# The last 512 tokens of a chained kernel: kept by token, stored by SyncE in place of GpSimd's indirect stores

## The chip, the cores and the metric

One core of a Trainium2 chip runs the whole kernel. The metric is the device time of one execution in microseconds; the median of three runs counts.

## What is computed

Three stages follow each other, each fed by the one before (B 4, H 8, S 768, D 48; 3072 tokens of 384 features):

```
# 1 linear attention with a decay for each key feature
for t in range(S):
    state = alpha[:, :, t, :, None] * state + einsum('bhd,bhe->bhde', k[:, :, t], v[:, :, t])
    y[:, :, t] = einsum('bhd,bhde->bhe', q[:, :, t], state)
x = y.transpose(0, 2, 1, 3).reshape(B * S, H * D)
# 2 each token goes through the one expert of 8 with the highest probability
logits = normed(x) @ normed(expert_emb).T / tau
expert_idx = argmax(logits, axis=1); gate_w = softmax(logits)[expert_idx]
for e in range(8):
    h = maximum(x[mask] @ w1[e], 0)              # 384 -> 1024
    out[mask] = gate_w[mask, None] * (h @ w2[e]) # 1024 -> 384
# 3 a dense network
h = x @ w_in                                     # 384 -> 2048
y = maximum(0.01 * h, h) @ w_out                 # 2048 -> 384
```

## The kernel before

The program is written by hand for the five engines. Each has its own list of instructions (`@block.sync`, `@block.gpsimd`, `@block.scalar`, `@block.vector`, `@block.tensor`), and semaphores order them. Nothing else sets an order: an engine does its instructions in the order written, and a wait holds back all that stands behind it on that engine.

**Attention** runs over 24 tiles of 128 tokens (6 chunks of each of the 4 batches, the batches in turn). SyncE stores each tile's result in the scratch tensor `x_rows` in memory (line 408).

**Routing.** VectorE works out, for every token, the expert and a place: the tokens are sorted by expert, and each expert's tokens begin a new block of 128 slots. 31 blocks (`WINDOWS`; "window" in the code) are enough for every split. Tables for the slots come out of it: `slot_src` (which token sits in a slot), `slot_gate` (its gate), `slot_dst` (the row of `y_rows` to which the slot's result goes), and `wtab`, a number for each block that tells the expert and when weights are to be split. `slot_dst` is worked out at lines 1093 to 1103, behind the splits of expert 0's weights and ahead of the block loop: it takes the empty slots out, so that `y_rows` holds the 3072 results without gaps, sorted by expert. Empty slots get a number beyond the rows and aren't written.

**The block loop** (`each_window`, 31 steps, two for each turn of a hardware loop, the last three written out). In step w TensorE does the hidden layer of block w+1, transposes the hidden values of block w (`hT`), transposes the gathered rows of block w+2 and contracts block w (line 1372). Every product of two fp32 operands is done as three matmuls on a high and a low part (`PARTS`): ScalarE copies the high part (`gxT`, `hT`, `wts`), VectorE subtracts it to get the low part (lines 1066, 1128, 375). VectorE scales the block's result by the gates into `ys` (line 1148), two buffers. GpSimd gathers block w+3's rows out of `x_rows` (line 578), copies the block's token numbers into column 384 of `ys` (line 598), copies its `slot_dst` (line 573), waits for `ys` and scatters the rows into `y_rows` by an indirect DMA (line 603). SyncE loads the next expert's weights (`load_expert`) each time a half of the buffer `raw` has been split.

**The second network** takes `y_rows` in 6 groups of 512 rows. SyncE loads a group in four DMAs, one for each 32 partitions (`load_y`, line 485), when the blocks that can hold its rows have been scattered; VectorE transposes it (line 1110), and TensorE does for each of 16 slices of 128 hidden features `inner` (line 1399) and `outward` (line 1434). ScalarE copies the four tiles of 128 results of a group to `os` (line 780, `o_copy`). As the rows are sorted by expert, the token number that stands beside each row is needed to store it: SyncE loads these numbers once (`tokens`, line 495), and GpSimd stores each tile by an indirect DMA to `out` (line 614), and waits for all stores at the end (line 618).

Each engine leaves the program through the end of the block; the records of this stand under line 64, where the block's context is opened.

## Time and profile before

| | before |
|---|---|
| median of 3 runs | 858.06 us |
| the runs | 859.18, 858.06, 854.04 us |
| the profiled execution | 856.75 us |
| its span, first to last instruction | 855.0 us |
| mean granted TensorE clock | 0.991 |
| TensorE busy (matmuls) | 833.1 us, 97% of the span |
| VectorE / ScalarE / GpSimd busy | 419.2 / 342.7 / 185.7 us |

The profiled execution is one of its own; 1.75 us of it lie outside the span. Attention takes up to about 122 us of the span, routing up to 144.8, the block loop up to about 443, the second network the rest.

### The profile page before, as it was taken

What the parts mean: (1) busy time and instruction counts of PE and PEld (TensorE: products, weight loads), DVE (VectorE), ACT (ScalarE), POOL (GpSimd) and SP (SyncE); (2) the same over time, 40 slices, a digit from 0 to 9 for tenths busy, and PEclk for the clock granted to TensorE, in tenths of its full rate; (3) what the DMA queues carried; (4) which work ended last, traced back from release to release, by engine and by line L of the source; (5) the groups of instructions that cost most, each with busy time, mean ns of one, the idle gap of its engine ahead of it and who ended that gap; (6) DMA issues with size and microseconds to landing.
All of it is one profiled execution on the core that took longest, in us unless ns stands there. A gap on an engine that the chain in (4) does not pass through costs nothing.

```text
span 855.0 us, 17220 instructions
## 1 busy us (share of the span) xinstructions
PE 833.1 (97%) x5554; PEld 751.6 (88%) x5555; DVE 419.2 (49%) x644; ACT 342.7 (40%) x663; POOL 185.7 (22%) x267
## 2 busy tenths in 40 slices
PE   7999999999999999999999999999999999999994
PEld 7888878999989999999999888898999888899993
DVE  7799969625444435445265433433533533433330
ACT  2455547535534435445254333333333323333231
POOL 6566624132223222232120001001001001001001
PEclk9899999999999999999999999999999999999997
DMA  9999761634335242396002201201201001001001
GB/s 211 230 220 222 185 213 56 223 113 163 140 110 193 76 148 102 115 242 205 24 3 38 38 1 38 37 1 37 37 0 37 0 0 38 1 1 37 1 1 37
DMA packets 46677, 76.38 MB, mean 89 GB/s; under 512 B 19559, under 2 KB 35987, under 8 KB 46640
## 3 DMA queue, kind: packets, MB, share of 16 engines
q1 hardware_dynamic: 40976, 60.30, 26.4%
q0 software_dynamic: 5504, 15.59, 5.2%
q8 instruction: 21, 0.34, 0.2%
q14 instruction: 16, 0.13, 0.0%
q10 hardware_dynamic: 160, 0.01, 0.0%
HBM read 61.68 MB, written 15.60 MB: 90 GB/s over the span
## 4 chain that ended last, share of the span: by engine, by line
PE 92%; DVE 2%; DMA 2%; POOL 1%; issue 1%; ACT 0%; SPq 0%; DVEq 0%; POOLq 0%; ACTq 0%
PE bank L1399 24%; PE bank L1434 23%; PE bank L1372 15%; PE bank L1352 15%; PE bank L1363 3%; PE bank L1236 2%; PE bank L1196 2%; PE bank L1213 2%; DMA qkas<-qka 2%; PE bank L1339 1%; PE bank L1244 1%; PE bank L1202 1%; PE bank L1256 1%; POOL kt L536 0%; PE bank L1187 0%
## 5 line engine op out<-in xcount | busy, mean ns | idle before, releaser
L1399 PE MATMUL bank<-yT,wts 128*128 128x512 f32 x864 | 217.0, 395 | 0.0
L1434 PE MATMUL bank<-wts,gs 128*128 128x384 f32 x1152 | 215.0, 334 | 0.0
L1434 PEld LDWEIGHTS bank<-wts,gs 128*128 128x128 f32 x1152 | 202.3, 188 | 8.9 <-issue 0.3
L1399 PEld LDWEIGHTS bank<-yT,wts 128*128 128x128 f32 x864 | 160.7, 188 | 30.7
L1162 DVE TENSOR_TENSOR g<-bank,small 128x512 f32<-128x512 f32 x96 | 66.4, 691 | 172.5 <-ACT small L789 172.5
L1352 PE MATMUL bank<-wts,gxT 128*128 (+1 forms) x558 | 141.5, 398 | 0.6 <-DVE gxT L1074 0.6
L1372 PE MATMUL bank<-wts,hT 128*128 x744 | 137.2, 339 | 0.0
L789 ACT ACTIVATE small<-bank 128x512 f32<-128x512 f32 x96 | 57.6, 600 | 187.5 <-PE bank L1399 180.0
L1372 PEld LDWEIGHTS bank<-wts,hT 128*128 128x128 f32 x744 | 128.5, 188 | 0.2
L1352 PEld LDWEIGHTS bank<-wts,gxT 128*128 128x128 f32 x558 | 101.9, 188 | 19.8 <-issue 0.8
L614 POOL DMA_INDIRECT out<-os,tokens x24 | 23.4, 973 | 377.0 <-ACT os L780 371.5
L1164 DVE TENSOR_TENSOR gs<-g,gs 128x512 fp32r<-128x512 f32 x96 | 66.6, 693 | 67.1 <-ACT gs L792 67.1
L792 ACT ACTIVATE gs<-g 128x512 fp32r<-128x512 f32 x96 | 60.7, 632 | 72.8 <-DVE g L1162 72.8
L748 ACT ACTIVATE hT<-bank 128x512 fp32r<-128x512 f32 x62 | 33.7, 597 | 123.9 <-PE bank L1363 123.9
L375 DVE TENSOR_TENSOR wts<-raw,wts 128x1024 f32 (+1 forms) x60 | 70.1, 1220 | 19.3 <-ACT wts L369 19.3
L603 POOL DMA_INDIRECT y_rows<-ys,idst x31 | 31.6, 1018 | 189.6 <-DVE ys L1148 189.6
L1128 DVE TENSOR_TENSOR hT<-bank,hT 128x512 fp32r<-128x512 f32 x62 | 39.9, 686 | 50.5 <-ACT hT L748 50.2
L369 ACT ACTIVATE wts<-raw 128x1024 f32 (+1 forms) x60 | 59.2, 1058 | 0.0
L1148 DVE TENSOR_SCALAR ys<-bank,slot_gate 128x384 f32<-128x384 f32 x31 | 19.0, 614 | 43.4 <-PE bank L1372 43.4
L720 ACT ACTIVATE hs<-bank 128x512 f32<-128x512 f32 x62 | 37.1, 599 | 4.9 <-PE bank L1352 4.9
L1066 DVE TENSOR_TENSOR gxT<-bank,gxT 128x384 fp32r<-128x384 f32 x30 | 16.7, 558 | 42.0 <-ACT gxT L716 42.0
L578 POOL DMA_INDIRECT xg<-x_rows,isrc x28 | 29.5, 1055 | 25.0 <-POOL isrc L573 24.1
(174 smaller groups left out, 732.9 us busy)
## 6 DMA issues: line engine op xcount, KB each, us to landing
raw<-w SPq DMA_DIRECT2D x14, 1536.0 KB, 7.0
qkas<-qka SPq DMA_DIRECT2D x40, 289.5 KB, 5.0
vs<-v SPq DMA_DIRECT2D x24, 192.0 KB, 4.9
x_rows<-xs SPq DMA_DIRECT2D x24, 192.0 KB, 4.4
yl<-y_rows SPq DMA_DIRECT2D x24, 192.0 KB
raw<-w_in SPq DMA_DIRECT2D x2, 1536.0 KB, 7.0
raw<-w_out SPq DMA_DIRECT2D x2, 1536.0 KB, 7.2
raw<-w SPq DMA_DIRECT2D x3, 512.0 KB, 4.0
```

The costliest lines, as they stand in the source:

```text
L369: act.activation(set_of(par, 0, cols), raw[:, cols], ACT.Copy).then_inc(w_hi, 1)
L375: dve.tensor_tensor(set_of(par, 1, cols), raw[:, cols], set_of(par, 0, cols).bitcast(F32), ALU.subtract).then_inc(w_lo, 1)
L720: act.activation(hs[:, u, half * HALF:(half + 1) * HALF], hps[u][half][:, :], ACT.Relu).then_inc(relu_done, 1)
L789: act.activation(small[:, f % 2], gps[f % 2][:, :], ACT.Copy, scale=0.01).then_inc(small_done, 1)
L792: act.activation(gs[:, f % 4, 0], g[:, f % 2], ACT.Copy).then_inc(g_hi, 1)
L1128: dve.tensor_tensor(hT[:, 1, h], htps[half][:, :], hT[:, 0, h].bitcast(F32), ALU.subtract).then_inc(ht_lo, 1)
L1162: dve.tensor_tensor(g[:, f % 2], gps[f % 2][:, :], small[:, f % 2], ALU.max).then_inc(g_done, 1)
L1164: dve.tensor_tensor(gs[:, f % 4, 1], g[:, f % 2], gs[:, f % 4, 0].bitcast(F32), ALU.subtract).then_inc(g_lo, 1)
L1352: m = pe.matmul(hps[u][half][:, :], gxT[:, u, x_part, k * P:(k + 1) * P], set_of(par, w_part, slice(n, n + HALF)), start=(k == 0 and (x_pa ...
L1372: m = pe.matmul(yeps, hT[:, h_part, k * P:(k + 1) * P], set_of(par, w_part, slice(n, n + D)), start=(k == 0 and (h_part, w_part) == (0, 0) ...
L1399: m = pe.matmul(gps[f % 2][:, :], wts[:, 0, w_part, n:n + P], yT[:, u, y_part, k], start=(k == 0 and (w_part, y_part) == (0, 0)), stop=(k ...
L1434: m = pe.matmul(ops[tt], gs[:, f % 4, g_part, tt * P:(tt + 1) * P], wts[:, 1, w_part, f * D:(f + 1) * D], start=(f == 0 and (g_part, w_par ...
```

## The change

The tokens of the last chunk of each batch, 4 tiles of 128, are called late (`LATE_TILES`: tiles 5, 11, 17 and 23 of the output). The other 2560 (`EARLY`) are treated as before: their rows lie in `y_rows` without gaps, sorted by expert, and make up groups 0 to 4. The late ones get the row `EARLY` + token, so that the scratch tensor has 5632 rows, of which the upper 3072 hold 512 that are written. Group 5 is loaded from those, tile by tile, so its rows are in the order of the output. SyncE then stores the four results of group 5 with plain DMAs, and waits for all stores in GpSimd's place.

`slot_dst` needs more for it: the count of early tokens of each expert (seven small operations, `kept` to `back_by`, between two splits of expert 0's weights), and for every slot whether it is late (`place_slots`, eleven operations, in VectorE's first block, behind the low part of block 2). VectorE's first two blocks are written out ahead of its loop (`each_window(dve, step, 1)`). GpSimd's wait for `slot_dst` moves into the step, behind the gather. The diff leaves out the new tiles and the new semaphore, the shape of `tokens` (20 columns), a condition in `wait_scattered` that leaves out a wait for nothing in blocks 0 and 1, and the size of the scratch tensor.

```diff
@@ -56,10 +56,15 @@
     YW = y_dram.shape[1]
-    assert YW == D + 4
-    y_blk = y_dram[:, 0:D].rearrange("(g n r) (j d) -> g j r n d", r=SQ, j=QUADS, n=GT // SQ)
-    y_token = y_dram[:, D:YW].rearrange("(t p) d -> p t d", p=P)
+    EARLY, LATE_TILES = N - GT, [b * CH + CH - 1 for b in range(BATCHES)]
+    Y_ROWS = EARLY + N
+    assert YW == D + 4 and y_dram.shape[0] == Y_ROWS and TG == BATCHES
+    y_blk = y_dram[0:EARLY, 0:D].rearrange("(g n r) (j d) -> g j r n d", r=SQ, j=QUADS, n=GT // SQ)
+    y_late = y_dram[EARLY:, 0:D].rearrange("(t n r) (j d) -> t j r n d", r=SQ, j=QUADS, n=P // SQ)
+    y_token = y_dram[0:EARLY, D:YW].rearrange("(t p) d -> p t d", p=P)
+    o_rows = out.rearrange("(t p) d -> t p d", p=P)
@@ -333,9 +341,11 @@
-        def each_window(eng, step):
-            with eng.Fori(0, WINDOWS // 2 - 1) as i:
+        def each_window(eng, step, apart=0):
+            for w in range(2 * apart):
+                step(w, w % 2, True, True)
+            with eng.Fori(apart, WINDOWS // 2 - 1) as i:
                 for u in range(2):
@@ -475,13 +486,18 @@
-                newest = min(t * TG + TG - 1 + E - 1, WINDOWS - 1)
+                newest = min(t * TG + 2 * TG - 1 + E - 1, WINDOWS - 1)
                 for j in range(2):
                     sp.wait_ge(scattered[j], 16 * ((newest + 2 - j) // 2))
                 if t >= 2:
                     sp.wait_ge(yt_turned, (t - 1) * KD)
                 for j in range(QUADS):
+                    if t == GROUPS - 1:
+                        for tt, tile in enumerate(LATE_TILES):
+                            sp.dma_start(yl[j * SQ:(j + 1) * SQ, u, tt * P // SQ:(tt + 1) * P // SQ],
+                                         y_late[tile, j]).then_inc(yl_in[u], 16)
+                        continue
                     sp.dma_start(yl[j * SQ:(j + 1) * SQ, u],
@@ -495,6 +511,12 @@
                 load_y(t, t % 2)
+            for tt, tile in enumerate(LATE_TILES):
+                sp.wait_ge(o_copied, (GROUPS - 1) * TG + tt + 1)
+                sp.dma_start(o_rows[tile], os_[:, 1, tt]).then_inc(late_stored, 16)
+            for u, s in enumerate(stored):
+                sp.wait_ge(s, 16 * TG * (GROUPS // 2 - u))
+            sp.wait_ge(late_stored, 16 * TG)
@@ -586,7 +608,6 @@
             pool.wait_ge(id_space, 1)
-            pool.wait_ge(tables_ready, 3)
@@ -595,6 +616,7 @@
                 wait_scattered(pool, w, u, pool_turns)
+                pool.wait_ge(tables_ready, 3)
                 pool.tensor_copy(ys[:, u, D:D + 1].bitcast(I32), slot_src[:, ds(w, 1)]).then_inc(idx_copied, 1)
@@ -602,20 +624,18 @@
                     out=y_dram, out_offset=bass.IndirectOffsetOnAxis(ap=idst[:, u:u + 1].bitcast(U32), axis=0),
-                    in_=ys[:, u, :], in_offset=None, bounds_check=N - 1, oob_is_err=False).then_inc(scattered[u], 16)
+                    in_=ys[:, u, :], in_offset=None, bounds_check=Y_ROWS - 1, oob_is_err=False).then_inc(scattered[u], 16)
             each_window(pool, step)
             pool.wait_ge(tokens_in, 16)
-            for t in range(GROUPS):
+            for t in range(GROUPS - 1):
                 for tt in range(TG):
                     n = t * TG + tt
                     pool.wait_ge(o_copied, n + 1)
                     pool.indirect_dma_start(
                         out=out, out_offset=bass.IndirectOffsetOnAxis(ap=tokens[:, n, 0:1].bitcast(U32), axis=0),
                         in_=os_[:, t % 2, tt], in_offset=None, bounds_check=N - 1, oob_is_err=False).then_inc(stored[t % 2], 16)
-            for s in stored:
-                pool.wait_ge(s, 16 * TG * (GROUPS // 2))
@@ -1034,8 +1054,6 @@
             tok, clear, empty, far, ghi = (slot_val[:, j, :] for j in range(5))
-            more = exp8[:, 6, 0:E - 1]
-            start("side", dve.tensor_tensor(more, base[:, 1:E], base[:, 0:E - 1], ALU.subtract))
             dve.wait_ge(slots_summed, 1)
@@ -1087,26 +1105,29 @@
             split_lo(dve, 0, 0, range(3, 4))
+            kept, kept_sum, kept_from, back, limit, back_by, limit_by = (exp_early[:, j, :] for j in range(7))
+            start("main", dve.tensor_tensor(kept, incl[:, :, TILES - TG - 1], starts, ALU.subtract))
+            after("main")
+            start("main", dve.tensor_tensor_scan(kept_sum, kept, zeros[:, 0:E], 0.0, ALU.add, ALU.add))
+            start("side", dve.scalar_tensor_tensor(out=limit, in0=cx, scalar=float(P), in1=kept, op0=ALU.mult, op1=ALU.add))
+            after("main")
+            start("main", dve.tensor_tensor(kept_from, kept_sum, kept, ALU.subtract))
+            after("side")
+            start("side", dve.tensor_tensor(limit_by[:, 0:E - 1], limit[:, 1:E], limit[:, 0:E - 1], ALU.subtract))
+            after("main")
+            start("main", dve.scalar_tensor_tensor(out=back, in0=cx, scalar=float(P), in1=kept_from,
+                                                   op0=ALU.mult, op1=ALU.subtract))
+            after("main")
+            start("main", dve.tensor_tensor(back_by[:, 0:E - 1], back[:, 1:E], back[:, 0:E - 1], ALU.subtract))
             gx_rest(1, 1)
             split_lo(dve, 0, 0, range(4, PIECES))
-            start("main", dve.tensor_tensor(wexp[:, :, 0:E - 1], wexp[:, :, 0:E - 1],
-                                            more.unsqueeze(1).to_broadcast([P, W, E - 1]), ALU.mult))
-            after("main")
-            start("main", dve.tensor_reduce(far, wexp[:, :, 0:E - 1], AX.X, ALU.add))
-            after("main")
-            start("main", dve.tensor_tensor(far, slot_row[:, :], far, ALU.subtract))
-            after("main")
-            start("main", dve.tensor_tensor(far, far, empty, ALU.add))
-            after("main")
-            dve.wait_ge(tables_ready, 2)
-            dve.tensor_copy(slot_dst[:, :], far).then_inc(tables_ready, 1)
             dve.wait_ge(gate_ready, 1)
             def y_turn(t, u, k):
                 if k == 0:
-                    dve.wait_ge(yl_in[u], (t - u) * 8 * QUADS + 16 * QUADS)
+                    loads = QUADS * (t // 2 + (TG if t == GROUPS - 1 else 1))
+                    dve.wait_ge(yl_in[u], 16 * loads)
                 dve.transpose(yf[:, (u * KD + k) % 2].rearrange("p (n r) -> p n r", r=SQ),
@@ -1114,6 +1135,39 @@
+            def place_slots():
+                def by_window(ap):
+                    return ap[:, 0:E - 1].unsqueeze(1).to_broadcast([P, W, E - 1])
+                back_w, limit_w, is_late = far, ghi, tok
+                after("main")
+                after("side")
+                start("main", dve.tensor_tensor(by_win[:, :, :], wexp[:, :, 0:E - 1], by_window(back_by), ALU.mult))
+                start("side", dve.tensor_tensor(wexp[:, :, 0:E - 1], wexp[:, :, 0:E - 1], by_window(limit_by), ALU.mult))
+                after("main")
+                start("main", dve.tensor_reduce(back_w, by_win[:, :, :], AX.X, ALU.add))
+                after("side")
+                start("side", dve.tensor_reduce(limit_w, wexp[:, :, 0:E - 1], AX.X, ALU.add))
+                after("main")
+                start("main", dve.tensor_tensor(back_w, slot_row[:, :], back_w, ALU.subtract))
+                after("side")
+                start("side", dve.scalar_tensor_tensor(out=is_late, in0=slot_row[:, :], scalar=limit[:, 0:1], in1=limit_w,
+                                                       op0=ALU.subtract, op1=ALU.is_ge))
+                after("main")
+                start("main", dve.scalar_tensor_tensor(out=clear, in0=clear, scalar=float(EARLY), in1=back_w,
+                                                       op0=ALU.add, op1=ALU.subtract))
+                after("side")
+                start("side", dve.tensor_tensor(back_w, back_w, empty, ALU.add))
+                after("main")
+                start("main", dve.tensor_tensor(clear, clear, is_late, ALU.mult))
+                after("side")
+                after("main")
+                start("main", dve.tensor_tensor(far, far, clear, ALU.add))
+                after("main")
+                dve.wait_ge(tables_ready, 2)
+                dve.tensor_copy(slot_dst[:, :], far).then_inc(tables_ready, 1)
@@ -1129,6 +1183,8 @@
                     gx_rest(w + 2, u)
+                if isinstance(w, int) and w == 0:
+                    place_slots()
                 with dve.If(late > 0):
@@ -1147,7 +1203,7 @@
-            each_window(dve, step)
+            each_window(dve, step, 1)
```

## How the change moves instructions

VectorE ahead of the block loop, before, from the last operation of the table `wtab` on (`exp` is the tile `exp8` with the experts' numbers, `squares` holds the slots' flags by expert, `slot_val` the slots' values):

```order
L1088 CAST wtab<-wflag 1x31
L375 TENSOR_TENSOR wts<-raw,wts 128x1024
L1066 TENSOR_TENSOR gxT<-bank,gxT 128x384
L375 TENSOR_TENSOR wts<-raw,wts 128x1024 x2
L1093 TENSOR_TENSOR squares<-squares,exp 128x31x7
L1096 TENSOR_REDUCE slot_val<-squares 128x31
L1098 TENSOR_TENSOR slot_val<-slot_row,slot_val 128x31
L1100 TENSOR_TENSOR slot_val<-slot_val 128x31
L1103 CAST slot_dst<-slot_val 128x31
L338 UNCONDITIONAL_BRANCH
```

and after:

```order
L1106 CAST wtab<-wflag 1x31
L386 TENSOR_TENSOR wts<-raw,wts 128x1024
L1109 TENSOR_TENSOR exp_early<-incl,exp 128x8
L1111 SCALAR_TENSOR_TENSOR exp_early<-exp_early,zeros 128x8
L1112 SCALAR_TENSOR_TENSOR exp_early<-exp,exp_early 128x8
L1114 TENSOR_TENSOR exp_early<-exp_early 128x8
L1116 TENSOR_TENSOR exp_early<-exp_early 128x7
L1118 SCALAR_TENSOR_TENSOR exp_early<-exp,exp_early 128x8
L1121 TENSOR_TENSOR exp_early<-exp_early 128x7
L1084 TENSOR_TENSOR gxT<-bank,gxT 128x384
L386 TENSOR_TENSOR wts<-raw,wts 128x1024 x2
L356 TENSOR_LOAD wtab
```

The seven operations on `exp_early` now stand ahead of block 1's low part (`gxT`), and the five that gave `slot_dst` are gone from ahead of the loop.

VectorE in block 0, after; before, the first three rows were followed by the branch to the weights' splits:

```order
L1182 TENSOR_TENSOR hT<-bank,hT 128x512 x2
L1084 TENSOR_TENSOR gxT<-bank,gxT 128x384
L1147 TENSOR_TENSOR by_win<-squares,exp_early 128x217
L1148 TENSOR_TENSOR squares<-squares,exp_early 128x31x7
L1150 TENSOR_REDUCE slot_val<-by_win 128x31
L1152 TENSOR_REDUCE slot_val<-squares 128x31
L1154 TENSOR_TENSOR slot_val<-slot_row,slot_val 128x31
L1156 SCALAR_TENSOR_TENSOR slot_val<-slot_row,exp_early,slot_val 128x31
L1159 SCALAR_TENSOR_TENSOR slot_val<-slot_val 128x31
L1162 TENSOR_TENSOR slot_val<-slot_val 128x31
L1164 TENSOR_TENSOR slot_val<-slot_val 128x31
L1167 TENSOR_TENSOR slot_val<-slot_val 128x31
L1170 CAST slot_dst<-slot_val 128x31
```

Eleven operations up to `slot_dst` now stand between block 2's low part and the splits of expert 1's weights.

The end of the list of SyncE before, with the waits:

```order
L485 DMA yl<-y_rows 32x16x96 [waits yt_turned,scattered1,scattered0]
L485 DMA yl<-y_rows 32x16x96 x3
L64 UNCONDITIONAL_BRANCH
```

and after:

```order
L498 DMA yl<-y_rows 32x4x96 [waits yt_turned,scattered1,scattered0]
L498 DMA yl<-y_rows 32x4x96 x15
L516 DMA out<-os 128x384 [waits o_copied] x4
L69 UNCONDITIONAL_BRANCH [waits late_stored,stored1,stored0]
```

and the end of GpSimd's, before and after:

```order
L614 DMA out<-os,tokens 3072x384 [waits o_copied,tokens_in]
L614 DMA out<-os,tokens 3072x384 [waits o_copied] x23
L64 UNCONDITIONAL_BRANCH [waits stored1,stored0]
```

```order
L636 DMA out<-os,tokens 3072x384 [waits o_copied,tokens_in]
L636 DMA out<-os,tokens 3072x384 [waits o_copied] x19
L69 UNCONDITIONAL_BRANCH
```

Four stores and the wait for all stores have gone from GpSimd to SyncE, and the last group's four loads have become sixteen.

## Rows read from the trace of the kernel before

**Rows 1.** The page: busy time, and the chain's shares by engine

```profile
PE 833.1 (97%) x5554; PEld 751.6 (88%) x5555; DVE 419.2 (49%) x644; ACT 342.7 (40%) x663; POOL 185.7 (22%) x267
PE 92%; DVE 2%; DMA 2%; POOL 1%; issue 1%; ACT 0%; SPq 0%; DVEq 0%; POOLq 0%; ACTq 0%
```

**Rows 2.** Chain of waits at the end: start us, us, what

```profile
842.38 0.50 ACT os L780
...
844.88 0.98 POOL out L614
```

**Rows 3.** Records of the program's end: count, duration ns, start us

```profile
L64 SPq DRAIN  x1: 122/122/122, 612.1 to 612.1; - x1
L64 PEldq DRAIN  x1: 3342/3342/3342, 839.0 to 839.0; - x1
...
L64 POOLq DRAIN  x1: 7098/7098/7098, 847.7 to 847.7; - x1
L618 POOLq EVENT_SEMAPHORE  x1: 17/17/17, 847.5 to 847.5; - x1
```

**Rows 4.** GpSimd, order of time: its last store of group 4

```profile
784.79 0.98 POOL L614 DMA_INDIRECT out<-os,tokens  x1 [0.30 <-issue]
```

**Rows 5.** Chain of waits, TensorE in blocks 0 and 1

```profile
147.47 4.16 PE bank L1352 x18
...
154.90 4.19 PE bank L1372 x24
...
164.44 4.19 PE bank L1372 x24
```

**Rows 6.** SyncE's stores of x (line 408): all 24, then the one at 119.6

```profile
DMA to landing us min/median/max: 1.8/4.4/7.6
...
L408 SPq DMA_DIRECT2D x_rows<-xs x1: 344/344/344, 119.6 to 119.6; - x1
DMA to landing us min/median/max: 1.9/1.9/1.9
```

**Rows 7.** VectorE, order of time, ahead of and in block 0

```profile
148.19 0.56 DVE L1066 TENSOR_TENSOR gxT<-bank,gxT 128x384 fp32r<-128x384 f32 x1 [0.99 <-ACT gxT L716]
...
150.94 0.38 DVE L1093 TENSOR_TENSOR squares<-squares,exp 128x217 f32<-128x217 f32 x1
...
151.76 0.19 DVE L1098 TENSOR_TENSOR slot_val<-slot_row,slot_val 128x31 f32<-128x31 f32 x1
...
152.22 0.18 DVE L1103 CAST slot_dst<-slot_val 128x31 int32<-128x31 f32 x1
...
155.46 0.56 DVE L1066 TENSOR_TENSOR gxT<-bank,gxT 128x384 fp32r<-128x384 f32 x1 [0.46 <-ACT gxT L716]
157.13 3.50 DVE L375 TENSOR_TENSOR wts<-raw,wts 128x1024 f32 x3 [1.11 <-ACT wts L369]
160.55 0.61 DVE L1148 TENSOR_SCALAR ys<-bank,slot_gate 128x384 f32<-128x384 f32 x1
162.28 1.29 DVE L1128 TENSOR_TENSOR hT<-bank,hT 128x512 fp32r<-128x512 f32 x2 [1.12 <-ACT hT L748]
```

**Rows 8.** GpSimd's gathers, and TensorE's first transposes of a gathered block

```profile
140.25 1.28 POOL L578 DMA_INDIRECT xg<-x_rows,slot_src  x1 [1.75 <-issue]
...
143.62 0.33 PEld L1332 LDWEIGHTS bank<-ident,xg 128*128 128x128 f32 x3 [0.19 <-DMA xg<-x_rows,slot_src]
...
164.20 1.06 POOL L578 DMA_INDIRECT xg<-x_rows,isrc  x1 [0.91 <-POOL isrc L573]
```

**Rows 9.** The loads of y_rows and the transposes of what they bring

```profile
L485 SPq DMA_DIRECT2D yl<-y_rows x24: 302/488/2817, 371.4 to 611.6; - x24
L1110 DVE STREAM_TRANSPOSE yf<-yl x18: 669/704/711, 431.0 to 743.2; 128x512 f32<-128x512 f32 x18
```

**Rows 10.** A gap of TensorE and the clock granted behind it

```profile
23.02 0.77 PE L1202 MATMUL bank<-ident,kt 112*128 112x112 f32 x4 [1.52 <-ACT knat L640]
...
28.00:30.00 2.00, 2.00 (x30) 1.91 (x28) 1.37 (x2) 1.67 (x5) 0.52 (x1) 0.50 1.03 258
```

More of the change, by code:

```diff
@@ L129, in build @@
             slot_row = sb("slot_row", [P, WINDOWS])
+            by_win = sb("by_win", [P, WINDOWS, E - 1])
+            exp_early = sb("exp_early", [P, 7, E])
             token1 = sb("token1", [P, TILES])
@@ L184, in build @@
             os_ = sb("os", [P, 2, TG, D])
-            tokens = sb("tokens", [P, TILES, YW - D])
+            tokens = sb("tokens", [P, TILES - TG, YW - D])
             small = nc.alloc_sbuf_tensor_at("small", [P, 2, GT], F32, offset=xg_at)
@@ L282, in build @@
         o_copied = sem("o_copied")
+        late_stored = sem("late_stored")
         stored = [sem(f"stored{j}") for j in range(2)]
@@ L356, in wait_scattered @@
             if isinstance(w, int):
-                eng.wait_ge(scattered[u], 16 * (w // 2))
+                if w > 1:
+                    eng.wait_ge(scattered[u], 16 * (w // 2))
             else:
@@ L1520 @@
     args = [nc.dram_tensor(n, a.shape, mybir.dt.from_np(a.dtype), kind="ExternalInput").ap() for n, a in arrays.items()]
-    scratch = [nc.dram_tensor(n, (B * S, w), F32).ap() for n, w in (("x_rows", H * HD), ("y_rows", H * HD + 4))]
+    scratch = [nc.dram_tensor(n, (rows, w), F32).ap()
+               for n, rows, w in (("x_rows", B * S, H * HD), ("y_rows", 2 * B * S - 512, H * HD + 4))]
     out = nc.dram_tensor("out", (B * S, moe2_w_out.shape[1]), F32, kind="ExternalOutput").ap()
```

## The prediction

> **What bounds the kernel now.** I read the page first. TensorE (PE) is busy 97% of the span [rows 1], at a mean granted clock of 0.991. Then the chain of waits: 92% of it is PE, and in the block loop and the second network one matmul stands directly behind the other. In the block loop the contractions of blocks 0 and 1 start at 154.90 and 164.44 us, so a block takes 9.55 us [rows 5]. So between 147.5 us and the last matmul at 842.4 us nothing done on another engine costs time unless it makes TensorE wait. Time can be won before or after that stretch.
>
> After it there is a lot. The chain [rows 2] shows the last copy out of PSUM (ScalarE, line 780) from 842.38, right behind the last matmul, to 842.88, and then GpSimd working off its queue: an indirect store takes it 0.98 us and 0.31 us pass before the next, so the stores that were ready at 840.3 to 842.9 are issued up to 844.88. Its wait for them ends at 847.5 (line 618, [rows 3]). The chain stops there, since what follows is no work, but the span goes on to 855.0. The records of the program's end [rows 3] say what fills it: each engine that leaves the program does a DRAIN and then meets the others. SyncE did its own at 612.1 (0.12 us), TensorE's ended with its last matmul. GpSimd's starts at 847.7 and lasts 7.10 us, to 854.8, and the span ends at 855.0. **7.1 of the 12.1 us behind the last copy are this one record**, and it begins only when GpSimd has nothing left to do.
>
> **The change, part by part.**
>
> *The last four stores go from GpSimd to SyncE.* Everything GpSimd still has to do in the second network is then its store of group 4, whose last issue is at 784.79 [rows 4], 58 us before the last copy. It no longer waits for stores either (SyncE does), so its DRAIN starts near 785.8 and, if it again takes 7.1 us, is over at 793, beneath group 5's matmuls. The new end is SyncE's: the last copy ends at 842.88, and the direct store starts 0.05 us later. The nearest rows for its price are the 24 stores of x (line 408), same engine, same 128 rows of 1.5 KB: 1.8 to 7.6 us to landing, median 4.4. The long ones have loads of q, k and the weights beside them; the one at 119.6, with little ahead of it, took 1.9 [rows 6]. At 842.9 only the store issued half a microsecond earlier is beside it, so I take 2.0 and keep 7.6 as the other end. Then leaving the program, 0.2 as GpSimd needed between its wait and its DRAIN, SyncE's DRAIN 0.12 [rows 3] and the meeting 0.2. Sum: 842.93 + 2.0 + 0.2 + 0.12 + 0.2 = 845.45, against 855.0: **9.55 us less**. Of that 2.45 us are the queue and landing of the indirect stores and 7.1 are the DRAIN.
>
> A rule speaks against the larger part. The row gives GpSimd's DRAIN at the program's end 7,098 ns against 122 ns for SyncE's [rows 3]. The Trainium skill, "VectorE: DVE Perf Modes", section "The DRAIN you can't avoid", holds the DRAINs of the preamble and postamble to be about 12 ns, constant, on all five engines. By it this record would be nothing that a kernel can move, and the change would be worth only the 2.45 us. The trace disagrees with the figure, so I go by the row. What the 7.1 us consist of, no row says.
>
> *Seven small operations on the experts' numbers (lines 1109 to 1121 after) ahead of block 1's low part.* In the trace of before VectorE is idle 0.99 us just there, waiting for ScalarE's high part [rows 7] (the row at 148.19). Five of the seven hang on each other at about 0.2 us each (two steps of 31-wide operations lie between 151.76 and 152.22, 0.23 each), the other two slip between: about 1.1 us, against the 0.99 idle. The low part ends at 148.75 or 0.1 later, and TensorE wants it when half of the 18 matmuls from 147.47 are done, at 149.55 [rows 5]: hidden, with 0.7 us to spare. If this cover is gone, each microsecond over costs one.
>
> *The slots' places go from ahead of the block loop into block 0.* Five operations (150.94 to 152.40, [rows 7]) leave a place at which VectorE then waits for ScalarE anyway: gain nothing. In block 0, behind the low part that ends at 156.02, eleven now run. Four are 217 wide (0.41 us from start to start: two lie between 150.94 and 151.76), seven 31 wide (0.23); two chains interleave, so I follow the longer one: 2.4 us. At the dearest, with no overlap, 4 x 0.41 + 7 x 0.32 = 3.9 us. Queued behind them on VectorE: the three splits of expert 1's first weights (start 157.13), the scaled rows of block 0 (160.55) and block 1's hT (162.28). With 2.4 us and 0.25 for the branch, the splits start at 158.67 and the hT at 162.7, the first half ready at 163.4. TensorE needs it for the contraction at 164.44: 1.0 us to spare, so the cost is **0**; at 3.9 us it is 0.5. Below nothing it can't be, since TensorE has no gap here to give back. In block 1 VectorE is idle over 1 us ahead of both its operations and has caught up.
>
> *GpSimd's wait for the places moves behind the gather of block 3.* That gather runs some 5 us earlier, needed by nobody before 164. Behind the wait stand block 0's two index copies, its scatter and the gather of block 4. The scatter follows the rows, 1.55 us later than now, so the gather goes from 164.20 to 165.75; the first gather needed 3.4 us until its transposes (140.25 to 143.62), so it is there at 169.2, and TensorE asks half a microsecond ahead of block 2's contraction at 173.99 [rows 5, 8]. Cost 0.
>
> *Groups' loads wait for four blocks more, and the last group comes in 16 loads.* Groups 0 and 1 now want blocks 14 and 18, where they wanted 10 and 14. Block 18 is contracted by 154.9 + 18 x 9.55 + 4.2 = 331 and stored some 5 us later, and the loads start at 371.4, held back by the weights ahead of them [rows 9]. Later groups are loaded after all blocks anyway. The last group's four loads are issued by 611.6, and the last of its three transposes starts at 743.2 [rows 9], so the first not before 730: even at the slowest issue there, 2.8 us, sixteen take 45 us of some 120. Cost 0. The larger scratch (5632 rows) is neither filled nor read whole.
>
> So the profiled execution, 856.75 us, becomes 847.2. The three runs shown have a median of 858.06, so by that 848.5; the profiled one lies within their spread of 5 us. I forecast **848.0**, between the two.
>
> **The rivals.**
>
> *The 7.1 us stay at the end.* GpSimd's DRAIN might not be free to finish until the whole program's transfers are over. For it: the record is 58 times SyncE's and starts just after GpSimd's last transfer landed, so it isn't a wait for that transfer, and what it waits for is not seen. Against: it is the only engine's DRAIN that is long without work in flight, and TensorE's, 3.34 us, ended exactly with TensorE's own work, which speaks for a DRAIN that looks at its own engine alone. Then the end is 844.93 + 0.2 + 7.1 + 0.2 = 852.4 and the median 858.06 - 2.6 = 855.5. This is also the time by the skill's rule above.
>
> *SyncE's stores land late.* Four stores within 2.6 us, at the price of the x stores in company: 4.4 to 7.6 us in place of 2.0, giving 851 to 854. Against: before, in the same place, the four indirect ones (the same bytes) landed within 2.6 us of their issue.
>
> *Block 0 becomes VectorE's, and it ends slower than before.* The new straight code (two blocks unrolled, 106 rows more) could stall VectorE, by fetching its code for instance. From 3.4 us for the places on, TensorE waits for hT. A gap of 1.52 us ahead of 23.0 us was followed by half clock (1.2 of 2.4 GHz) that still stood in the stretch from 28 to 30 [rows 10]; 7 us at half speed cost 3.5 us more. The kernel is slower than before once the gap is over 6 us: a stall of 8 us would give 858.06 - 9.55 + 8 + 3.5 = 860. In the trace VectorE runs some 80 straight-line instructions ahead of the loop with hardly a gap. A gap of 1 to 3 us would give 849.5 to 855.
>
> **How the numbers follow.** The forecast 0.77; the 7.1 us stay 0.11; late landing 0.05; a small gap in block 0 0.04; slower than before 0.03. The forecast's own range, with the spread of a median of few runs, is 845 to 851.5. To hold 8 in 10 the range must take in part of the middle cases, to 853.5, and leaves out the DRAIN that stays. A change of 1% (8.6 us) is about what a measurement of this kernel can tell; the forecast of 9.55 lies just over it, and the bound is at 849.5. Faster by over 1%: three quarters of the forecast's 0.77, 0.57; within 1%: the rest of it and the other cases, 0.40; slower 0.03.
>
> **What the profile after would show.** Right: GpSimd's DRAIN near 786, SyncE's the last, the span ending within 3 us of the last copy, the last matmul still at 842.4. Eleven operations between 156 and 158.5 on VectorE, no TensorE gap at 164.4. Wrong: a long DRAIN of any engine behind 845, landings over 3 us on line 516, a gap on TensorE in blocks 0 or 1, or group 5's transposes waiting for loads.

## The result

| | before | changed |
|---|---|---|
| median of 4 runs | 856.27 us | **844.78 us** |
| the runs | 854.04 to 859.18 | 844.51 to 845.98 |
| ratio, 95% interval | | 0.9867 (0.9829 to 0.9904) |
| the profiled execution, its span | 856.75, 855.0 us | 845.98, 844.2 us |
| mean granted clock | 0.991 | 0.997 |

Faster by 1.3%, 11.5 us by these medians. The forecast was 848.0 us with a range from 845.0: the time came out 0.2 us below the range. Part of the 11.5 us is the luck of few runs: over more runs, below, the change is worth 9.6 us.

The page of the changed kernel, busy time and the chain's shares, against [rows 1]:

```profile
PE 832.2 (99%) x5554; PEld 750.9 (89%) x5555; DVE 420.6 (50%) x656; ACT 342.4 (41%) x663; POOL 184.7 (22%) x263
PE 93%; DVE 2%; DMA 2%; POOL 1%; issue 1%; ACT 0%; SPq 0%; DVEq 0%; POOLq 0%; ACTq 0%
```

TensorE has the same work (832.2 us busy against 833.1) in a shorter span. The chain of waits at the end, against [rows 2]:

```profile
835.05 6.29 PE bank L1490 x36
...
841.35 0.49 ACT os L800
```

No GpSimd stands in it any more; it ends with ScalarE's last copy at 841.84. The records of the program's end (count, duration in ns, start in us), against [rows 3]:

```profile
L69 POOLq DRAIN  x1: 10143/10143/10143, 781.4 to 781.4; - x1
...
L69 PEldq DRAIN  x1: 3335/3335/3335, 838.0 to 838.0; - x1
...
L69 SPq COMPARE_BRANCH  x1: 38/38/38, 843.9 to 843.9; - x1
L69 SPq DRAIN  x1: 7/7/7, 844.0 to 844.0; - x1
L69 SPq EVENT_SEMAPHORE  x1: 17/17/17, 844.2 to 844.2; - x1
```

GpSimd's DRAIN is still the longest, 10.1 us even, but it begins at 781.4, since its sequencer gets there while GpSimd still works off its last stores, and is over at 791.5, beneath group 5. SyncE's last store lands, it leaves at 843.9, and 0.3 us later all are let go. The span goes on 2.4 us behind the last copy, where it was 12.1: **9.76 us of the 10.8 between the two spans**. GpSimd's last store and SyncE's four (duration, landing), against [rows 4, 6]:

```profile
783.77 0.97 POOL L636 DMA_INDIRECT out<-os,tokens  x1 [0.30 <-issue]
...
L516 SPq DMA_DIRECT2D out<-os x4: 332/347/362, 839.3 to 841.9; - x4
DMA to landing us min/median/max: 1.9/1.9/1.9
```

1.9 us to landing each. The chain in blocks 0 and 1, against [rows 5]:

```profile
146.42 4.17 PE bank L1408 x18
...
153.87 4.18 PE bank L1428 x24
...
163.42 4.19 PE bank L1428 x24
```

All of it stands 1.0 us earlier than before, and the contractions are 9.55 us apart as before: no gap came in. VectorE, against [rows 7]:

```profile
146.09 0.15 DVE L1109 TENSOR_TENSOR exp_early<-incl,exp 128x8 f32<-128x8 f32 x1
...
146.88 0.17 DVE L1121 TENSOR_TENSOR exp_early<-exp_early 128x7 f32<-128x7 f32 x1
147.14 0.56 DVE L1084 TENSOR_TENSOR gxT<-bank,gxT 128x384 fp32r<-128x384 f32 x1
...
154.43 0.56 DVE L1084 TENSOR_TENSOR gxT<-bank,gxT 128x384 fp32r<-128x384 f32 x1 [1.45 <-ACT gxT L736]
154.91 0.38 DVE L1147 TENSOR_TENSOR by_win<-squares,exp_early 128x217 f32<-128x217 f32 x1
...
157.09 0.18 DVE L1170 CAST slot_dst<-slot_val 128x31 int32<-128x31 f32 x1
157.68 3.50 DVE L386 TENSOR_TENSOR wts<-raw,wts 128x1024 f32 x3 [0.41 <-issue]
161.09 0.61 DVE L1204 TENSOR_SCALAR ys<-bank,slot_gate 128x384 f32<-128x384 f32 x1
161.62 1.28 DVE L1182 TENSOR_TENSOR hT<-bank,hT 128x512 fp32r<-128x512 f32 x2
```

The seven operations take 0.97 us and the low part behind them starts 1.05 us earlier than before, which is the shift of everything: they cost nothing. The eleven take 2.36 us, the splits start 3.25 us behind the start of block 2's low part (1.67 before), and block 1's hT starts at 161.62, at once when the rows are scaled; its first half is ready at 162.3 for the contraction at 163.42. GpSimd's order and SyncE's loads of group 5, against [rows 8, 9]:

```profile
147.68 2.06 POOL L600 DMA_INDIRECT xg<-x_rows,isrc  x1 [0.89 <-POOL isrc L595]
157.43 0.18 POOL L620 COPY ys<-slot_src 128x1 int32 x1 [7.70 <-DVE slot_dst L1170]
...
162.62 1.02 POOL L625 DMA_INDIRECT y_rows<-ys,idst  x1 [4.88 <-DVE ys L1204]
...
164.74 1.06 POOL L600 DMA_INDIRECT xg<-x_rows,isrc  x1 [0.90 <-POOL isrc L595]
...
609.19 7.42 SPq L498 DMA_DIRECT2D yl<-y_rows  x16
```

The gather of block 3 goes ahead of the wait, the scatter of block 0 and the gather of block 4 come later, and the sixteen loads take 7.4 us, over 100 us before anyone wants them.

The 1.0 us that isn't the end was there before TensorE's first block: it is attention's (sixteen matmuls near its end start at 113.57 us against 114.61). In both profiles TensorE waits at 21.5 us for a copy of ScalarE that stands behind the wait for the next chunk's loads, and has half clock for some microseconds behind it; the changed kernel's gap was 1.2 us against 1.5 in [rows 10], and its clock back at 28 us against 30. The change touches nothing there, and after_again, below, shows that the 1.0 us isn't its work.

### The profile page after: what moved, and what is told of

Read it like the earlier page. It is cut to its first block, busy times and chain, and to the rows that moved or that the text cites. A ratio compares the mean times of both kernels' runs of the same rounds, so it can differ in the third digit from the quotient of the medians.

```text
span 844.2 us, 17203 instructions
## 1 busy us (share of the span) xinstructions
PE 832.2 (99%) x5554; PEld 750.9 (89%) x5555; DVE 420.6 (50%) x656; ACT 342.4 (41%) x663; POOL 184.7 (22%) x263
## 4 chain that ended last, share of the span: by engine, by line
PE 93%; DVE 2%; DMA 2%; POOL 1%; issue 1%; ACT 0%; SPq 0%; DVEq 0%; POOLq 0%; ACTq 0%
PE bank L1455 24%; PE bank L1490 24%; PE bank L1428 15%; PE bank L1408 15%; PE bank L1419 3%; PE bank L1252 2%; PE bank L1292 2%; DMA qkas<-qka 2%; PE bank L1269 2%; PE bank L1300 1%; PE bank L1395 1%; PE bank L1258 1%; PE bank L1312 1%; POOL kt L558 1%; PE bank L1243 0%
## 5 line engine op out<-in xcount | busy, mean ns | idle before, releaser
L636 POOL DMA_INDIRECT out<-os,tokens x20 | 19.5, 973 | 320.8 <-ACT os L800 316.2
```

## The experiments

The ratios are to runs of the kernel before on the same chip, with 95% intervals.

**before_again: no edit.**

> The kernel before, unchanged, for its spread. Theory base: its runs differ (854.0 to 859.2 so far) by what happens in attention, where TensorE's granted clock falls to half for some microseconds in the profile (mean clock 0.991); runs with a mean clock near 1.0 should take 854 to 855 us, those at 0.991 or below 856 to 859. Rival: the spread has nothing to do with the clock, and runs of equal clock differ by 4 us.

854.54 us (12 runs, 853.48 to 857.22), ratio 1.0007 (0.9994 to 1.0020). Together with the 20 runs beside it, the 23 runs of a mean clock of 0.994 or more took 852.8 to 855.5 us, the 9 of 0.990 to 0.993 took 855.7 to 857.3. Its profile had a short gap, and the clock kept (the last row is block 0's contraction in the chain, 2.6 us earlier than in [rows 5]):

```profile
22.62 0.60 PE L1202 MATMUL bank<-ident,kt 112*128 112x112 f32 x4 [0.57 <-ACT knat L640]
...
28.00:30.00 2.00, 2.00 (x38) 1.89 (x38) 2.00 (x3) 0.72 (x3) 1.79 (x2) 1.00 1.08 312
...
152.27 4.20 PE bank L1372 x24
```

So these two profiles differ by the length of that gap and by what the clock does behind it, and the theory holds for these 32 runs. In the 26 runs of this kernel beside the later ones it is less clean: one at 0.994 took 856.48 us. The 0.995 that remains is the end of the program: TensorE idle at half clock for 8 to 9 us is 0.5% of the span.

The gap and the clock can be set side by side in ten profiles, all those in which ScalarE's copies stand behind the wait. Where the gap that ends between 21.7 and 23.9 us was 0.18 to 0.92 us (late_by_gpsimd, before_again, places_slow, places_ahead, sync_waits), the clock stayed full from 20 to 32 us; where it was 1.22 to 1.81 us (after, after_third, before, after_again, gpsimd_waits), it fell to half. But it isn't the only place where the clock falls: in places_slow it was half for some microseconds between 40 and 48 us. What followed for the forecast is below: **the median of 20 runs of the kernel before is 854.18, not 858.06** (854.70 of 17 and 855.56 of 9 beside the later kernels).

**after_again, after_third: no edit.**

> The changed kernel, unchanged. Theory: 9.8 us of its gain are the program's end (12.1 us behind the last copy before, 2.4 after), in every run; the rest is the clock in attention. So at equal mean clock this kernel is 9.5 to 10 us faster than the one before, and the ratio lies at 0.986 to 0.989. Rival: the change also makes attention itself quicker, and at equal clock the difference is over 11 us.

844.62 us (844.37 to 846.95), ratio 0.9882 (0.9868 to 0.9896). Against 854.18 this is 9.56 us. Three of its runs have a clock of 1.000 and took 844.4 to 844.8, as did the three such runs of the first set (844.5 to 844.8). The runs of the kernel before at 0.995 or more, with nothing lost but at the end, have a median of 854.06: 9.5 us between them. The theory holds, and the rival (attention itself quicker) falls. (The 1.000 of the changed kernel stands against 0.995, not against 1.000, because the long idle end is gone.)

> The changed kernel again, beside the next one on the same chip, since seed_later was run on another chip than after_again and its runs (845.1 to 846.1) can't be set beside 844.4 to 847.0. Theory: median 844.5 to 845.6, and one run in some four 1.5 us or more above the fastest.

845.00 us (844.09 to 847.44), ratio 0.9876 (0.9854 to 0.9898): the median is as expected, and two runs of the five lie over 1.5 us above the fastest, where one in four was expected. The difference to the kernel before is 10.6 us here, not 9.6: four of the nine runs of that kernel beside it, whose median is 855.56, had a clock of 0.992 or less.

**gpsimd_waits: GpSimd leaves late, with nothing to do.**

```diff
                         in_=os_[:, t % 2, tt], ...).then_inc(stored[t % 2], 16)
+            pool.wait_ge(o_copied, GROUPS * TG)
```

> The changed kernel, with one wait more: GpSimd, after its last indirect store (group 4), waits for the last copy of group 5 before it leaves the program. It moves no data there. Theory one (the DRAIN is the price of leaving, whenever GpSimd does it): its DRAIN starts at about 842 and takes 7 us again, so the kernel ends at about 849, 5 us slower than the changed kernel. Theory two (the DRAIN clears up after the last indirect transfers, and time passed counts): nothing is left to do 55 us later, the DRAIN takes under 0.5 us and the time is that of the changed kernel within 0.5 us.

851.30 us (850.52 to 851.91), ratio 0.9958 (0.9944 to 0.9973). The DRAINs (duration in ns, start in us), two of the program's start and two of its end:

```profile
L1576 SPq DRAIN  x1: 7/7/7, 0.3 to 0.3; - x1
L1576 POOLq DRAIN  x1: 188/188/188, 0.4 to 0.4; - x1
...
L69 POOLq DRAIN  x1: 6772/6772/6772, 843.2 to 843.2; - x1
L69 SPq DRAIN  x1: 7/7/7, 845.2 to 845.2; - x1
```

Theory one holds: 57 us after its last store was issued GpSimd's DRAIN takes 6.77 us, from 843.2 to 850.0, and the kernel ends there; SyncE was done at 845.2. The span goes on 7.2 us behind the last copy, where the changed kernel's has 2.4: 4.8 us, as theory one said (5). The median is 6.7 us above the changed kernel's. The other 1.9 us aren't the end's: this profile had the longest gap at 22 us (1.81 us) and half clock behind it, and the four runs' clocks of 0.993 to 0.996 are lower than the end alone makes them. Why all four were so, no run shows.

So the 7 us aren't work left over from the last stores, for they didn't wear off in 57 us. They stand at GpSimd's leaving the program and count when it leaves last. They aren't the price of any DRAIN either: at the program's start GpSimd's took 0.19 us (183 to 189 ns in all twelve profiles), before it had issued a transfer. What in between makes the difference, the transfers it has issued or something else, is open.

**sync_waits: the kernel before, the final wait moved.**

```diff
-            for s in stored:
-                pool.wait_ge(s, 16 * TG * (GROUPS // 2))
...
+            for s in stored:
+                sp.wait_ge(s, 16 * TG * (GROUPS // 2))
```

> The kernel before, where only the final wait for the stores is moved from GpSimd to SyncE; GpSimd still issues all 24 indirect stores, the last at about 844.9, and then leaves. Theory one (the DRAIN runs from when GpSimd is done issuing and takes some 7 us): it is over at about 853, and the kernel gains 1.5 to 2 us on the one before. Theory two (it takes until some 7 us after the last transfer has landed): no gain, 0 to 0.5 us. In both the 9.8 us of the change need GpSimd's stores to go, not only its wait.

852.18 us (851.13 to 853.15), ratio 0.9973 (0.9963 to 0.9984): 2.0 us for one moved wait, as theory one said (by the ratio 2.3).

```profile
L64 POOLq DRAIN  x1: 9487/9487/9487, 841.7 to 841.7; - x1
L64 SPq DRAIN  x1: 7/7/7, 845.9 to 845.9; - x1
```

The record starts at 841.7, while GpSimd still has two stores to issue (the last from 843.10 to 844.08), and ends at 851.2, 7.1 us behind them. In the changed kernel it was 6.8 us, from 784.7 to 791.5. The record covers GpSimd's work on its own queue and then these 7 us. They run from the last issue and not from the last landing, which SyncE had seen before 845.7, so theory two falls. The span goes on 10.3 us behind the last copy, where it was 12.1 to 12.2.

**late_by_gpsimd: the changed kernel, its last four stores plain, but GpSimd's.**

```diff
+            for tt, tile in enumerate(LATE_TILES):
+                pool.wait_ge(o_copied, (GROUPS - 1) * TG + tt + 1)
+                pool.dma_start(o_rows[tile], os_[:, 1, tt]).then_inc(late_stored, 16)
...
-            for tt, tile in enumerate(LATE_TILES):
-                sp.wait_ge(o_copied, (GROUPS - 1) * TG + tt + 1)
-                sp.dma_start(o_rows[tile], os_[:, 1, tt]).then_inc(late_stored, 16)
```

> The changed kernel (late tokens by token, places in block 0), but its last four stores are plain DMAs that GpSimd issues; SyncE only waits. It tells the part of the order of the rows from the part of the engine. Theory (the DRAIN runs from the end of GpSimd's own list and takes about 7 us): it starts at about 843 and ends at 850 or later, so the kernel takes 851 to 853 us, 7 to 8 more than the changed one, although no indirect store is left at the end. Rival (only indirect stores make it long, the plain ones don't): 845 to 846 us.

850.81 us (849.36 to 853.20), ratio 0.9950 (0.9933 to 0.9966). GpSimd's last plain store, and its DRAIN:

```profile
840.63 1.07 POOL L638 DMA_DIRECT2D out<-os  x2 [0.91 <-ACT os L800]
...
L69 POOLq DRAIN  x1: 7675/7675/7675, 841.1 to 841.1; - x1
```

The theory holds: with plain stores, SyncE's wait and the tokens in order GpSimd's DRAIN still ends the kernel (at 848.8 in the profile), and it is about 6 us slower than the changed one (0.7% by the ratios). It came just below the 851 to 853 expected.

The order by token isn't worth nothing, though. With it the stores are plain, GpSimd issues one in 0.54 to 0.60 us where an indirect one took 0.97 and 0.3 between two, and no queue is left at the end: the span goes on 8.2 us behind the last copy, against 10.3 in sync_waits. So in the profiles the 9.8 us split into about 1.8 for the wait, 2.1 for plain stores and 5.8 for the other engine. Whether another engine could issue the indirect stores as they were, no run tried.

**places_ahead: place_slots ahead of the block loop.**

```diff
-                if isinstance(w, int) and w == 0:
-                    place_slots()
...
-            each_window(dve, step, 1)
+            place_slots()
+            each_window(dve, step)
```

> The changed kernel with place_slots back ahead of the block loop, and VectorE's blocks not written out. My prediction held the move to be worth nothing in itself. Eleven operations of 2.4 us there end at about 152.4 us in the time of the profile after, and block 0's hT would start at 153.6, its first half ready at 154.3, where TensorE wants it at 153.87: a gap of about 0.4 us, so the place in block 0 is worth 0.4 us for the longer chain. Rival: VectorE runs its register work ahead, hT starts at 152.9 and there is no gap.

846.21 us (845.20 to 847.34), ratio 0.9896 (0.9865 to 0.9927). VectorE's last operation of the places and block 0's hT, then TensorE's 18 matmuls of a hidden layer ahead of it and its contractions of blocks 0 and 1:

```profile
150.35 0.18 DVE L1170 CAST slot_dst<-slot_val 128x31 int32<-128x31 f32 x1
151.86 1.29 DVE L1182 TENSOR_TENSOR hT<-bank,hT 128x512 fp32r<-128x512 f32 x2 [1.33 <-issue]
```

```profile
144.45 4.42 PE L1407 MATMUL bank<-wts,gxT 128*128 128x512 f32 x18
...
152.81 4.44 PE L1427 MATMUL bank<-wts,hT 128*128 x24 [0.66 <-DVE hT L1182]
...
162.36 2.87 PE L1427 MATMUL bank<-wts,hT 128*128 x15
```

A gap of 0.66 us, where I expected 0.4 (the way from the last operation into the first hT takes 1.33 us, the table's load and the branches, and wasn't run ahead: the rival falls). The gap costs more than its length: from the 18 matmuls' start at 144.45 to block 1's contraction at 162.36 it is 17.91 us, and 16.99 in the changed kernel (146.18 to 163.17). The time can't tell 0.9 us from none by its interval; the rows can. The place in block 0 is worth 0.9 us for the longer chain.

**places_slow: 2.5 us more on VectorE in block 0.**

```diff
+                for _ in range(6):
+                    start("main", dve.tensor_tensor(by_win[:, :, :], wexp[:, :, 0:E - 1], by_window(back_by), ALU.mult))
+                    after("main")
                 start("main", dve.tensor_tensor(by_win[:, :, :], wexp[:, :, 0:E - 1], by_window(back_by), ALU.mult))
```

> The changed kernel with six more operations of 217 elements in a chain ahead of the places' own (their results aren't used), 6 x 0.41 = 2.5 us more in block 0. The profile after shows block 1's first low half of hT ready at 162.3 us and wanted at 163.42, 1.1 us to spare. Theory: TensorE gets a gap of 1.4 us ahead of block 1's contraction, the kernel takes 1.4 us more and the clock stays. Rival: the gap is followed by half clock, as after the gap at 22 us, and it costs 3 us or more. Other rival: no gap, since something else covers it.

848.62 us (846.36 to 850.33), ratio 0.9911 (0.9878 to 0.9943). TensorE's contraction of block 1:

```profile
167.18 4.43 PE L1431 MATMUL bank<-wts,hT 128*128 x24 [1.66 <-DVE hT L1185]
```

and in the chain the contractions of blocks 1 and 2:

```profile
167.18 4.43 PE bank L1431 x24
...
177.37 4.19 PE bank L1431 x24
```

A gap of 1.66 us where 1.4 was expected, so 1.1 us was the slack within 0.3. The granted clock stayed full from 160 to 180 us, so the rival with half clock falls. But the next contraction comes 10.19 us behind this one and not 9.55, so the gap costs 2.3 us, 0.6 more than its length. The fastest run, 846.36, is 2.0 and 2.3 us above the fastest of after_again and after_third. The rest of the 3.6 to 4.0 us on the median is in part the clock: two of the four runs had 0.996 and 0.998, and the profile, which is one of them, has 0.94 in the stretch from 32 to 60 us.

**seed_later: ScalarE's wait for the loads behind its copies.**

```diff
+                late_seed = is_first(c) and b == 1
-                if within(three[0]):
+                if within(three[0]) and not late_seed:
                     seed(*three)
...
+                if late_seed:
+                    seed(*three)
```

> The changed kernel, where ScalarE in one step of attention (chunk 0, batch 1) does its wait for the next chunk's loads behind its four copies and not ahead of them. In the profiles it stands in that wait from 16.2 to 22 or 23 us, TensorE waits up to 1.8 us for the copies behind it, and in some executions its clock is then half for up to 7 us. Theory (this gap, of changing length with the loads, is what makes executions of one kernel differ by 1 to 3 us): no gap ahead of 23 us, mean clock 1.000 in all runs, and the slowest run comes down from 846 or 847 to about 844.5; the median falls by 0 to 0.5 us, since in the executions without the drop the loads and the scans behind them set the pace. Rival: the gap only moves, and the clock drops as before.

845.58 us (845.08 to 846.08), ratio 0.9885 (0.9862 to 0.9908). TensorE in its profile, and two stretches with the granted clock in the last column but two:

```profile
26.99 1.16 PE L1255 MATMUL bank<-qt,kt 48*128 48x128 f32 x16 [1.71 <-POOL kt L558]
...
26.00:28.00 2.00, 1.01 (x16) 0.97 (x16) 2.00 (x4) 1.90 (x6) 1.45 (x2) 1.00 1.08 216
28.00:30.00 2.00, 2.00 (x25) 1.80 (x23) 1.93 (x4) 0.27 (x2) 1.55 (x2) 1.00 0.99 238
```

> The kernel of seed_later again, beside the changed one. Its first profile had no gap at 22 us, but a gap of 1.7 us ahead of 27 us, where TensorE waits for GpSimd's kt behind the late loads. Theory (the gap only moves): median within 0.5 us of the changed kernel's, and the spread of its runs alike. Rival: lower by 0.5 us or more.

845.85 us (844.86 to 846.58), ratio 0.9881 (0.9862 to 0.9900), beside 845.00 for the changed kernel. The gap at 22 us is gone and another stands ahead of 27, where the same late loads are waited for by a longer way. The clock was 0.998 in four of the first six runs, so the theory of seed_later (1.000 in all) fails, and of its rival the first half holds: the gap moves. The second half isn't seen in the profiles. Behind the moved gap, 1.71 us in both, the clock stayed full; in seed_later_2's profile it was half at another place, from about 13 to 16 us:

```profile
14.00:16.00 2.00, 2.00 (x16) 1.70 (x18) 2.00 (x3) 0.64 (x2) 2.00 (x2) 0.50 1.01 263
```

The median is 0.85 us above the changed kernel's, outside the 0.5 of seed_later_2's theory and not the way of its rival, but well within the intervals. The spread may be smaller (1.0 and 1.7 us against 3.4), which is too few runs to say. It is no faster, and the changed kernel stays the best one.

## Why the forecast was nearly right, and where it failed

- **The end of the program: right.** Forecast 9.55 us less behind the last copy, measured 9.76. GpSimd's DRAIN went to 781 to 791, SyncE's store landed in 1.9 us (2.0 taken), and SyncE needed 0.01 us for its DRAIN, where I took 0.12; 0.2 for leaving was right.
- **The rule of the Trainium skill.** The Trainium skill, "VectorE: DVE Perf Modes", section "The DRAIN you can't avoid", gives about 12 ns on all five engines for the DRAINs that the runtime puts into preamble and postamble. The prediction read it as a rule on the records of line 64, which carry the line of the kernel's own block, so it may not be about them. At the program's start it comes near: 7 to 10 ns on four engines, but 0.19 us on GpSimd. At the end it doesn't: 7 ns for SyncE in the ten profiles in which it waits for the stores, but 122 ns in the two of the kernel before, 0.5 to 3.3 us for ScalarE, VectorE and TensorE, and 6.8 to 10.1 us for GpSimd in all twelve. Going by the row was right.
- **"The 7.1 us stay at the end", given 0.11: wrong.** gpsimd_waits and the profile of the changed kernel show what was open: the 7 us come when GpSimd leaves, while other engines still work, and don't wait for the whole program's transfers.
- **The seven and the eleven operations: right.** 0.97 us for 1.1, 2.36 for 2.4, both hidden. The slack in block 0 was put at 1.0 us, 1.1 was read afterwards, and places_slow confirmed it to 0.3. The gain of the place was put at 0; ahead of the loop, with eleven operations in place of five, they would have cost 0.9 us. "TensorE waits" was priced at the gap's length, and both gaps made here cost 0.3 and 0.6 us more than that.
- **GpSimd's order, the later loads, sixteen loads: right,** all hidden.
- **The base: wrong, and this is the step that failed.** "The three runs shown have a median of 858.06, so by that 848.5", and the forecast was set between this and the profiled execution's 847.2. Twenty more runs have a median of 854.18; less 9.55 that is 844.6, what the changed kernel takes beside them. The effect was forecast to 0.2 us, and the base was some 3 to 4 us off. The term that it left out is the clock in attention: between the profile before and before_again's, the same kernel, it and the gap ahead of it make 2.6 us (block 0's contraction at 154.90 and 152.27). The forecast from the profile, 847.2 against the 845.98 of the changed kernel's profiled execution, misses for the same reason: 1.0 of the 1.2 us is attention. With it **the range's low end** was wrong: it stood at 845.0 while one of the three runs, 854.04, less 9.55 already gives 844.5. The text put its range down to "the spread of a median of few runs" and didn't ask what made it, though the page showed a mean clock of 0.991 and [rows 10] where it fell; a profile with such a drop is a slow sample, not a middle one.
- The chance of 0.57 for faster by over 1% was about right for an effect of 1.12% (9.56 of 854.18) at a bound of 1%; the first measurement gave 1.3%, the two later ones 1.2%. Whether the time falls just below the range's end of 845.0 or on it is chance (844.78, 844.62 and 845.00 in the three sets of runs); the 3 us to the forecast aren't.

## What to carry to other kernels

The chain of waits ends with the last work, but the span doesn't: read the records of the program's end as well. If GpSimd leaves last, as here, look for a long DRAIN that no busy time shows (7 us in this kernel); give the last stores and the last wait to another engine and let GpSimd leave while others work (the wait alone gave 2 us here, the stores with it 9.6). And before forecasting an absolute time from three runs that differ by 0.6%, find what differs in them, and take the range from the fastest run too.

## What the runs showed of the hardware

- GpSimd's DRAIN at the program's end took 6.8 us, 57 us behind its last store, and 7.1 right behind landed stores; where its record begins with stores still in its queue it is longer (7.7 to 10.1) and ends 6.8 to 7.1 us behind the last of them. The other engines' is 0.007 to 0.12 us, or as long as their own last work. At the program's start GpSimd's took 0.19 us. What GpSimd does in it no row shows, and a program in which GpSimd issues no transfers at all wasn't tried.
- A direct store of 128 rows of 1.5 KB by SyncE landed in 1.9 us with little beside it, one by GpSimd in 2.2 to 2.4, an indirect one by GpSimd 2.6 us after its issue. GpSimd issued an indirect one each 1.28 us and a direct one in 0.56, SyncE a direct one in 0.35.
- TensorE kept its full clock through a gap of 1.66 us in the block loop, and had half clock behind gaps of 1.2 to 1.8 us at 22 us in attention, where matmuls are small and stand apart. But behind a gap of 1.71 us ahead of 27 and 28 us, in attention too, it kept it in both profiles. The gap's length alone doesn't decide it, and no run here shows what does.
- A gap in the block loop's matmuls cost more than its length: 0.66 us of idle time put the contraction behind it back by 0.9 us (places_ahead), 1.66 us by 2.3 (places_slow), at full clock.
